# One tile of the first MLP computed two heads earlier on TensorE, and its chain started one step sooner

## The reference

```python
# attention: 2 batches x 8 heads, 768 tokens, head size 64, 16 clusters
q_assign = argmax(normalised(q) @ normalised(centroids).T)
k_assign = argmax(normalised(k) @ normalised(centroids).T)
mask = q_assign[:, :, :, None] == k_assign[:, :, None, :]
scores = where(mask, (q @ k.T) / 8, -1e9)
attn = softmax(scores)
x = (attn @ v)                       # -> 1536 tokens x 512

# first MLP, 512 -> 2048 -> 512
h = x @ w_in
P = a[0] + a[1] * h + a[2] * h**2 + a[3] * h**3
Q = 1.0 + abs(b[0]) * abs(h) + abs(b[1]) * h**2
x = (P / (Q + 1e-6)) @ w_out

# second MLP, 512 -> 1536 -> 512
g = x @ w_gate
out = (g * sigmoid(g) * (x @ w_val)) @ w_out
```

## Time and profile before

| | us |
|---|---|
| median of 3 runs | 784.8 (784.11 to 784.89) |
| the profiled execution, its own time | 783.97 |
| its span in the profile | 782.2 |
| PE busy | 776.2 (99%) |
| POOL, DVE, ACT busy | 522.9, 569.8, 514.4 |

### The profile page before, as it was taken

The page is one execution under the profiler, slowest core; times in us unless marked ns, Lnnn a source line. Parts: engine busy times, 40 slices in busy tenths (PEclk is TensorE's granted clock), DMA queues, the critical chain, the costliest instruction groups (busy, mean ns, idle before and its releaser), DMA issues.

```text
span 782.2 us, 12708 instructions
## 1 busy us (share of the span) xinstructions
PE 776.2 (99%) x4247; PEld 702.5 (90%) x4247; DVE 569.8 (73%) x1047; ACT 514.4 (66%) x957; POOL 522.9 (67%) x457
## 2 busy tenths in 40 slices
PE   9999999999999999999999999999999999999998
PEld 8999999999998888888888888899999999999997
DVE  6999999999996888777776877654544545554454
ACT  5888888888886787777767789554544444333322
POOL 5678999998575898212222488879888975665620
PEclk9999999999999999999999999999999999999999
DMA  9685674644302600000000111342111113211102
GB/s 209 165 199 132 183 179 122 162 127 107 86 32 82 189 0 1 1 0 1 1 0 1 28 30 53 88 128 54 44 38 54 54 28 135 55 37 45 28 0 81
DMA packets 57682, 57.92 MB, mean 74 GB/s; under 512 B 6609, under 2 KB 44305, under 8 KB 57617
## 3 DMA queue, kind: packets, MB, share of 16 engines
q1 hardware_dynamic: 57376, 56.52, 27.0%
q10 hardware_dynamic: 240, 0.59, 0.3%
HBM read 33.59 MB, written 3.15 MB: 47 GB/s over the span
## 4 chain that ended last, share of the span: by engine, by line
PE 96%; DVE 1%; DMA 1%; ACT 1%; issue 0%; SPq 0%; ACTq 0%
PE ps L1225 19%; PE ps L1227 19%; PE ps L1226 19%; PE ps L1373 8%; PE ps L1390 4%; PE ps L1321 4%; PE ps L1322 4%; PE ps L1356 4%; PE ps L1320 4%; PE ps L1392 4%; PE ps L1359 4%; PE ps L1424 2%; DMA qk_low<-qk_hi 1%; DVE probT_lo L1147 0%; PE ps L1332 0%; DVE neg_max L1121 0%
## 5 line engine op out<-in xcount | busy, mean ns | idle before, releaser
L561 POOL TENSOR_TENSOR den<-den,mag 128x512 f32<-128x512 f32 x48 | 62.3, 1298 | 122.0 <-ACT den L741 121.8
L1227 PE MATMUL ps<-x_hi,w_lo 128*128 128x512 f32 (+1 forms) x384 | 139.5, 363 | 0.0
L620 POOL TENSOR_TENSOR w_lo<-w_raw,w_hi 128x768 fp32r<-128x768 f32 (+1 forms) x48 | 101.7, 2127 | 56.6 <-ACT w_hi L794 56.6
L1225 PE MATMUL ps<-x_hi,w_hi 128*128 128x512 f32 (+1 forms) x384 | 139.4, 363 | 0.0
L1226 PE MATMUL ps<-x_lo,w_hi 128*128 128x512 f32 (+1 forms) x384 | 139.3, 363 | 0.0
L639 POOL TENSOR_SCALAR prob<-prob,row_inv 128x768 f32<-128x768 f32 x96 | 85.7, 908 | 28.9 <-DVE row_inv L1137 27.9
L1147 DVE TENSOR_TENSOR probT_lo<-ps,probT_hi 128x384 fp32r<-128x384 f32 x192 | 97.5, 549 | 6.7 <-ACT probT_hi L882 5.7
L882 ACT ACTIVATE probT_hi<-ps 128x384 fp32r<-128x384 f32 x192 | 83.7, 489 | 26.5 <-PE ps L1373 25.3
L1121 DVE TENSOR_REDUCE neg_max<-ps 128x1 f32<-128x768 f32 x96 | 90.9, 948 | 0.7 <-PE ps L1359 0.5
L862 ACT ACTIVATE prob<-ps,neg_max 128x768 f32<-128x768 f32 x96 | 86.6, 903 | 1.4 <-DVE neg_max L1121 1.1
L1373 PE MATMUL ps<-ident,prob 128*128 128x128 f32 x576 | 79.8, 274 | 1.2 <-DVE probT_lo L1147 1.1
(11 more groups left out here) (147 smaller groups left out, 1992.3 us busy)
## 6 DMA issues: line engine op xcount, KB each, us to landing
k_hihi<-qk_hi SPq DMA_DIRECT2D x32, 192.0 KB, 4.1
w_raw<-in_moe_w_gate SPq DMA_DIRECT2D x48, 128.0 KB, 2.3
w_raw<-in_moe_w_val SPq DMA_DIRECT2D x48, 128.0 KB, 2.6
w_raw<-in_moe_w_in SPq DMA_DIRECT2D x16, 256.0 KB, 3.7
w_raw<-in_moe_w_out SPq DMA_DIRECT2D x16, 256.0 KB, 4.7
qk_raw<-in_q SPq DMA_DIRECT2D x16, 192.0 KB, 3.3
q_hilo<-qk_hi SPq DMA_DIRECT2D x16, 192.0 KB, 3.8
qk_low<-qk_hi SPq DMA_DIRECT2D x16, 192.0 KB, 4.5
```

Of the source, the lines that this page charges most:

```text
L620: did(g.tensor_tensor(lo[:, wave, :], raw[:, wave, :], hi[:, wave, :].bitcast(F32), ALU.subtract), s_w2lo)
L1225: mm(dst, hi, m_hi, start=start, stop=False)
L1227: return mm(dst, lo, m_hi, start=False, stop=stop)
```

## The change

The first hidden tile is computed in the two steps NT - 2 * T + 2 = 86 and NT - T + 2 = 92, between the scores and the turn, and goes to bank 7 in place of bank 0. The steps 96 to 103, which held tiles 0 to 3, now hold tiles 1 to 4; the main loop starts its hidden tiles at 5 in place of 4. The chain of tile 0 moves from step 98 to step 97, that of tile 1 from step 100 to step 99, and that of tile 2 from behind the steps into step 102; the finishes move from 99 and 101 to 98, 100 and (tile 2) 103. The number of instructions and transfers of every engine is the same, and SP's queue is unchanged. The new waits of `first_hidden` are for the last cluster ranking and, for tiles 1 to 4, for the exponentials that free banks 1, 2, 3 and 0.

```diff
@@ -198,6 +198,10 @@
     HID, RES = 0, 4
     OUT = 2
+
+    def hid_bank(n):
+
+        return HID + n % 4 if n else PREP
 
@@ -368,10 +372,11 @@
-    AHEAD = 4
-    TAIL_CHUNKS = {NT + n: ((2 * n) // DC, (2 * n) % DC) for n in range(AHEAD * DC // 2)}
-    TAIL = {NT + 2: 0, NT + 4: 1}
-    TAIL_LOG = {NT + 3: 0, NT + 5: 1}
+    AHEAD = 5
+    TAIL_CHUNKS = {NT - 2 * T + 2: (0, 0), NT - T + 2: (0, 2)}
+    TAIL_CHUNKS.update({NT + n: (1 + (2 * n) // DC, (2 * n) % DC) for n in range((AHEAD - 1) * DC // 2)})
+    TAIL = {NT + 1: 0, NT + 3: 1, NT + 6: 2}
+    TAIL_LOG = {NT + 2: 0, NT + 4: 1, NT + 7: 2}
 
@@ -733,7 +738,7 @@
-                    hid = ps[:, HID + n % 4, :]
+                    hid = ps[:, hid_bank(n), :]
                     s.activation(mag[i][:, :], hid, ACT.Abs).then_inc(s_mag, 1)
...
@@ -1241,15 +1246,17 @@
                     pe.wait_ge(s_xlo, H // 2 * batches)
-                if n < 4:
-                    pe.wait_ge(s_exp, NT - 1 + n // 2)
+                if n == 0:
+                    pe.wait_ge(s_cluster, 2 * (NH - 1))
+                elif n < 5:
+                    pe.wait_ge(s_exp, NT - 1 + n % 4 // 2)
                 if n < POOL_UNITS:
                     pe.wait_ge(s_w1p, n + 1)
                 elif n < NF1:
                     pe.wait_ge(s_w1lo, n - POOL_UNITS + 1)
-                if n >= 4:
+                if n >= 5:
                     pe.wait_ge(s_glo, n - 3)
-                last = hidden(HID + n % 4, w1_hi[u], w1_lo[u], n // NF1, chunks)
+                last = hidden(hid_bank(n), w1_hi[u], w1_lo[u], n // NF1, chunks)
```

More of the change, by code:

```diff
@@ L762, in hidden_finish @@
                         sc.wait_ge(s_y, n - 3)
-                    s.activation(g_hi[(n - 1) % 3][:, :], ps[:, HID + (n - 1) % 4, :], ACT.Copy
+                    s.activation(g_hi[(n - 1) % 3][:, :], ps[:, hid_bank(n - 1), :], ACT.Copy
                                  ).then_inc(s_ghi, 1)
@@ L777, in hidden_finish @@
                     sc.wait_ge(s_num2, n + 1)
-                    s.activation(ps[:, HID + n % 4, :], log_q[:, :], ACT.Exp, scale=-1.0).then_inc(s_inv0, 1)
+                    s.activation(ps[:, hid_bank(n), :], log_q[:, :], ACT.Exp, scale=-1.0).then_inc(s_inv0, 1)
                 if n == N1:
@@ L994, in mlps @@
                 if 1 <= n <= N1:
-                    i1, inv1 = (n - 1) % 2, ps[:, HID + (n - 1) % 4, :]
+                    i1, inv1 = (n - 1) % 2, ps[:, hid_bank(n - 1), :]
                     ve.wait_ge(s_inv0, n)
```

## The result

| | before | changed |
|---|---|---|
| median of 7 runs, us | 784.78 (783.97 to 785.34) | 786.43 (785.95 to 788.42) |
| ratio of the times | 1 | 1.0032, 95% interval 1.0022 to 1.0041 |
| the profiled execution, its own time, us | 783.97 | 788.23 |
| its span in the profile, us | 782.2 | 786.5 |

What follows compares the result with a forecast made beforehand. PE, busy for 99% of the span, was taken as the bound. The terms -1.64 + 0.9 + 2.3 + 1.3 - 0.2 - 0.2 gave +2.4 us, so 787.2 us against the 784.8 median; range 784.2 to 788.6.

Steps and rivals of the forecast that it cites:

- part 1: Steps 86 and 92: six matmuls of hidden tile 0 in each cover PE's waits for low parts; net -1.64 us.
- part 2: Turn of tile 94: tile 0 read a step sooner, its num operations delay DVE's low parts of tile 93; +0.9 us.
- part 3: First products of step 101: tile 1's chain on DVE precedes low(95) and the x sum; largest stall, +2.3 us.
- part 4: Third quarter of R0, tile 0's result: g_lo(1) stands ahead of the last x sum on DVE; +1.3 us.
- part 5: Small earlier PE waits, step 97 to R0 and R0 to hidden tile 6, vanish; -0.2 us each.
- what cost nothing: Weight unit 6's split for hidden tile 6, SP's later weight loads, the bank change and new `first_hidden` waits: costed at nothing.
- likeliest case: The forecast itself: all counted stalls occur, own range 786.2 to 788.3 us; chance 0.62.
- Fill only: Rival: the chain fits in steps 97 to 103 and only the fill remains; -1.8 us, 783.0 us, chance 0.13.
- Stalls overlap: Rival: stalls overlap, leaving only the one at step 101; +0.5 us, 785.3 us, chance 0.17.
- A late engine: Rival: unit 6's split or a load comes late by up to 2.1 us; up to 789.3 us, chance 0.05.
- The falling clock: Rival: PE's clock halves for a stretch as long as the 2.3 us wait; 1.1 us more, 788.3 us, chance 0.03.

Runs made afterwards that it cites:

- e6: Changed kernel with the chain of tiles 0 to 2 reordered, as single operations on ACT and DVE, within steps 97 to 103: 782.96 us, ratio 0.9982.
- e7: e6 without the fill: tile 0 back in steps 96 and 97 in bank 0, four tiles ahead: 784.23 us, ratio 0.9995.
- e2: Kernel before with the changed kernel's earlier chain steps, without the fill in steps 86 and 92: 789.52 us, ratio 1.0064.
- e3: Changed kernel with only g_lo of tiles 0 and 1 moved on DVE behind the x sums of steps 100 and 103: 784.73 us, ratio 1.0005.
- e5: Changed kernel with 12 matmuls of zeros ahead of the products of step 101: 787.17 us, ratio 1.0036.
- e8: The changed kernel itself run again, unaltered, which gave its second profile: 786.46 us, ratio 1.0032.
- e4: Changed kernel with only tile 0's two num operations moved on DVE to step 98, behind the low parts of tile 93: 788.98 us, ratio 1.0057.
- e1: Changed kernel keeping the fill in steps 86 and 92, but with the chain in the steps of the kernel before: 786.71 us, ratio 1.0029.

## Why the prediction was right

**The bound and the fill (part 1).** PE is the bound throughout, and the waits of steps 86 and 92 vanished, as the rows above show. Their worth was put at 1.64 us. Step 96's turn comes 1.16 us later than before in the second profile of the changed kernel (25.78 us behind the turn of step 85, against 24.62); forecast were 1.14. Twelve matmuls fewer give back 2.72 us, not 2.78, since those of the main loop are 0.227 us apart. e6 against e7 measured 1.2 to 1.3 us for the whole fill; the last 0.3 us is e6's own short wait for g_lo of tile 2, shown there, which the stalls of the changed kernel hide.

**The wait at turn 94 (part 2).** Predicted at 0.8, and 0.9 with the second half. Turn 93 to turn 94 took 243.99 - 240.43 = 3.56 us in place of 2.75: 0.81, and the turn is listed 0.1 us longer. The chain through ACT's read, DVE's num and low(93) came out at 243.29 for a forecast of 243.15, and 0.13 us of that is the start of the kernel.

**The wait ahead of step 101 (part 3).** Predicted at 2.3, with the products at 251.75 and the x sum at 251.1; they came at 251.90 and 251.19, and the listed wait is 2.15 us. e2 shows that the chain's steps cause it, e3 that g_lo in front of the low parts carries 0.65 us of it, and e6, which moves the rest of tile 1's chain behind the x sum as well, has no wait there.

**The wait within R0 (part 4).** Predicted at 1.3; R0's third quarter came 261.07 - 258.40 = 2.67 us after its start, 1.28 more than the 1.39 of before. e3 removes it by moving g_lo(1) alone.

**The vanished waits (part 5) and what cost nothing.** R1 and R2 run on without a listed wait. Hidden tile 6 was not held up by its weights: in the second profile the split of its unit ended at 266.05 + 2.41 = 268.46 us, 1.95 us ahead of it, where before it was 0.86. Neither term was tested by itself.

**The sum.** The terms add up to 2.46 us, stated as +2.4. The second profile of the changed kernel, with a full clock, follows them stage by stage. Lateness against before, counted from the turn of step 85:

| place | forecast | second profile |
|---|---|---|
| turn of step 96 | +1.14 | +1.16 |
| start of R0 | +4.1 | +4.21 |
| third quarter of R0 | +5.4 | +5.49 |
| hidden tile 6 | +2.46 | +2.51 |

The total is no meeting of errors that cancel. That the ratio of all runs also says +2.5 us (0.32%, interval 0.22 to 0.41%) is in part luck: it holds the runs in which the clock fell, which the sum did not count, 3 of 14. The median came at 786.43 us, 0.8 us under the forecast 787.2 and inside the likeliest case's range.

**The rivals.** "Fill only" fell: it needed the x sum of step 100 by 248.8, and it came at 251.19. "Stalls overlap" fell, since all three are there in full. A late engine did not show. The falling clock was given 0.03 and an extra 1.1 us. It does happen, in the first profiled execution, at a cost of 1.6 us, but only in some executions of this kernel, so it moved the upper end of the times and hardly the median. Its chance was too small, since a wait of over 2 us was itself forecast. Nor could tell that no earlier wait had done it: a 9 there stands for 90% or more of a slice of nearly 20 us, and the same line of the changed kernel's page is all nines too, with the fall in it. Stretches of 2 us have to be read; those of before show 1.00 from 250 to 266 us. The Trainium skill, TensorE: Matmul & The Clock Gate, section Why this matters for your kernels, warns against idle gaps between bursts of matmuls. The trace agrees in kind, with a clock of 0.56 to 0.58 behind a gap of 2.15 us. This gap is shorter than those that the page warns of, and for its length the measurement decides.

**What stays open.** The spread of about 1 us with a full clock, in e5 and e8 and before too (783.66 to 786.65 us over 23 runs); the profiles place some of it ahead of step 85. In the second profile of the changed kernel PE stands still for 0.48 and 0.31 us ahead of scores at 93.76 and 122.48 us, in e4 for 1.03 us at 108.42, and waits there for nothing that the profile shows; the first profile has no such gap. No run looked for the cause.

## What to carry to other kernels

Work that is put earlier into an engine's in-order program is only free if every operation of it is ready when it gets its turn: one that waits for another engine (here g_lo for g_hi, behind a copy) holds up all that stands behind it, and the bound engine pays. Follow each of the moved operations to what it waits for, and place the pieces singly, behind the work that the bound engine asks for. Moving a piece back is not safe by itself either: in e4 the wait came back larger through another engine's queue.

## What the runs showed of the hardware

Behind a long idle wait of PE in the middle of dense work, the clock of TensorE fell towards its lower level, 1.2 GHz, in some executions. I count a run as one in which it fell when its mean granted clock is 0.998 or less; 0.999 also occurs in the kernel before, which has no such wait.

| kernel | longest listed wait in these steps, us | runs in which the clock fell |
|---|---|---|
| e6, e7 | none | 0 of 22 |
| e5, with zeros | 0.73 ahead of step 101 (1.12 in R0) | 0 of 5 |
| e3 | 1.50 | 0 of 11 |
| changed kernel (with e8) | 2.15 | 3 of 14 |
| e2 | 2.15 | 2 of 5 |
| e1 | 2.55 | 5 of 7 |
| e4 | 3.06 | 5 of 5 |

The share grows with the wait. Why one execution with a wait of 2.15 us keeps its clock and another does not stays open. The slow stretch in e4 (columns as above):

```profile
252.00:254.00 2.00, 0.37 (x1) 0.40 (x2) 1.94 (x4) 1.97 (x4) 1.60 (x2) 0.84 1.00 290
254.00:256.00 2.00, 2.00 (x7) 1.81 (x7) 1.93 (x4) 0.36 (x1) 1.06 (x1) 0.50 0.72 238
256.00:258.00 2.00, 2.00 (x10) 1.72 (x9) 1.06 (x2) 0.00 (x0) 0.00 (x0) 0.81 0.01 3
```

So a wait of the bound engine of some 2 us can cost nearly twice its length, 2.2 + 1.6 us here, and in only some of the executions. With zeros multiplied in the wait the clock fell in none of five runs (e5), at no gain in the median; with the wait removed it fell in none of eleven (e6), and the kernel was faster.
